# A fused attention and mixture-of-experts kernel: seven smaller expert weight loads, a later first load, and the last rank sums two slots later

## Chip, cores and metric

The kernel runs on one core of a Trainium2 chip. The metric is the device time of one execution in microseconds (us). KB are 1024 bytes.

## What is computed

The reference, cut to what matters:

```python
# 1. attention with decay, per batch and head; 3072 tokens of 384 = 8 heads x 48
for t in range(S):
    cur = einsum('bhd,bhe->bhde', u[None] * k[t], v[t])
    y[t] = einsum('bhd,bhde->bhe', r[t], state + cur)
    state = w * state + einsum('bhd,bhe->bhde', k[t], v[t])
# 2. dense layer, 384 -> 2048 -> 384
h = x @ w_in
x = (h * sigmoid(h)) @ w_out
# 3. eight experts, 384 -> 1024 -> 384; each token goes to one of them
e_idx = argmax(x @ w_gate + modality_bias[modality_id], axis=1)
gate_w = softmax(...)[e_idx]
for e in range(8):
    mask = e_idx == e
    out[mask] = gate_w[mask, None] * (maximum(x[mask] @ w1[e], 0) @ w2[e])
```

## The kernel before

All matrix products are done in three passes: each operand is split into a high and a low part (`_hi`, `_lo`, type float32r), and high x high, high x low and low x high are summed in PSUM. ScalarE makes the high parts (a cast), VectorE the low parts (a subtraction).

**Attention and dense stage.** `whole_block` writes out the program of every engine. The attention is cut into 48 units ("quads", u). The dense layer works on 12 tiles of 256 tokens; each has 16 *slots* f, one for every 128 of the 2048 inner features. In slot F = 16 t + f TensorE does the up step of f (`up_step`, nine matmuls, which raises `h_made`) and the down step of three slots before (`down_step`, six matmuls); the attention units are put into the slots by tables. The slots 0 to 2 of a tile have no down step of their own, since the tile before finished with them. In the last dense tile (t = 11, slots 176 to 191; F0 is 176) the first work for the experts is mixed in: `tensor_last_tile` transposes the gathered tokens of expert tile 0 in slot 3 (`turn`, L566 to L571, six transposes L570, waiting for `x_gathered`), `scalar_last_tile` makes the high parts of the first w1 in slots 8 to 11 and of the first w2 in slots 12 to 15, and `vector_last_tile` the low parts behind them.

**Expert stage.** Tokens are sorted by expert through lists in device memory. An expert tile is 256 tokens of one expert, and with these inputs there are 13 of them. In `tensor_experts` a tile has 8 up steps (nine matmuls each, L591 to L593), the down products of its first 128 tokens (8 x 3 matmuls, L618 to L620), the `turn` of the next tile's tokens, and the down products of the other 128 tokens. Tiles 0 and 1 are written out, the others run in a loop. In tile 0, VectorE chooses the experts of the last 512 tokens and counts them behind slot 1 (`route_choose`, `route_count`, L471 to L473); TensorE sums the ranks behind slot 3 (L595 to L601, waits for `lists_ready`); VectorE does the gates, takes the ranks and starts the tile table behind slots 4 to 6 (L474 to L485). At the end of tile 0 it computes the places, and GpSimd scatters the entries into the lists (L406 to L410).

**Weights.** An expert's w1 (128 x 3 x 1024, 1536 KB) goes to `raw1` and its w2 (128 x 8 x 384, 1536 KB) to `raw2`, each as one DMA from SyncE (`sync_load1`, `sync_load2`, L313 to L319). Each partition reads 12 KB in one piece. `raw1`, `raw2` and `x_in` lie in the buffer `store`, so the first load waits for the last attention unit (`y_done`). In SyncE's program the first load (`sync_first`) stands at slot 176, then the write of the tokens of dense tile 10 to `x_rows` (L896, waits for ScalarE's `copy_rows` in slots 0 and 1 of the last tile), then `sync_second` and the rest. A buffer is loaded again when the low parts have been made from it (`w1_lo_made`, `w2_lo_made`). The high and low parts of w2 lie in the first 8 rows of the dense layer's `wo_hi` and `wo_lo`, whose rows are 392 wide; 384 are used.

**GpSimd** (`pool_experts`) loads the list of the next tile (L989 for the first, then L358), gathers its tokens (L995 for the first, then L371, two indirect DMAs), and writes results out (L388, two indirect DMAs). Before it overwrites `entries_out` (L375), which ScalarE needs for the scales of the next results, it waits until the results written have landed.

## Time and profile before

| | |
|---|---|
| median of 3 runs | 782.63 us (782.56 to 784.86) |
| profiled execution, its time | 785.89 us |
| profiled execution, span | 784.3 us |
| TensorE busy | 743.2 us (95%) |
| VectorE, ScalarE, GpSimd busy | 501.8, 421.4, 235.0 us |
| mean granted clock of TensorE | 0.98 |
| DMA | 104.95 MB, mean 134 GB/s |
| last dense tile | about 501 to 540 us |
| expert tiles | about 540 to 774 us |

The profile is of one execution; times in it are from the start of its span. PE is TensorE's matmuls, PEld its weight loads, DVE VectorE, ACT ScalarE, POOL GpSimd, SP (SPq) SyncE. Engine clocks are given as a share of 2.4 GHz. A row of the windows view has the stretch and its length, the busy time (and number of instructions) of PE, PEld, DVE, ACT and POOL, the granted clock, the busy share of the DMA engines and GB/s. A row of a timeline has start, duration, engine, line, operation, output and inputs, and in brackets the idle time before it with what ended it. Matmuls overlap: each is shown with its whole passage, and the next starts before it ends (two up-step matmuls start about 0.12 us apart and take 0.28 each). "issue" as a releaser means that the view found no instruction that released the waiting one. Tiles that lie in the buffer `store` have its name in the rows (raw1, raw2, x_in); w1's parts are shown as wi_hi and wi_lo, w2's as wo_hi and wo_lo, and the experts' h likewise as wi_hi and wi_lo. in_w is w1 or w2 in device memory.

### The profile page before, as it was taken

To read this page: it belongs to the slowest core of one execution; us is meant where nothing else is said; L and a number is where in the kernel's file an instruction comes from. 1 tells how busy PE (TensorE), PEld (TensorE's weight loads), DVE (VectorE), ACT (ScalarE), POOL (GpSimd) and SP (SyncE) were. 2 spreads that over 40 slices of the span, in tenths; PEclk is the share of its full clock that TensorE was granted. 3 is DMA by queue.
4 is the path that set the end of the run, shared out by engine and by line. 5 is a ranking of instruction groups with operands and counts; after the bars stand their busy time and mean duration, and the time that the engine had idled before them with its cause. 6 is when DMAs were issued, how large, how long until landed. Compare 5 with 4: busy or idle time off the path is not lost.

```text
span 784.3 us, 24913 instructions
## 1 busy us (share of the span) xinstructions
PE 743.2 (95%) x9894; PEld 723.8 (92%) x9894; DVE 501.8 (64%) x1348; ACT 421.4 (54%) x1076; POOL 235.0 (30%) x349
## 2 busy tenths in 40 slices
PE   3599999999999999999999999899998999999994
PEld 3598899999999999999999999899998999999994
DVE  7889765856585666655676657245874766566662
ACT  4776555555453645555554554354563755566552
POOL 4531222332124222422133212210423334434431
PEclk9599999999999999999999999999999999999997
DMA  8941222222122222221222210505465755666561
GB/s 313 399 172 39 95 76 94 78 61 85 64 97 76 95 77 96 75 82 59 91 76 96 76 59 2 202 21 181 133 229 182 262 201 210 238 241 232 199 218 66
DMA packets 24160, 104.95 MB, mean 134 GB/s; under 512 B 4411, under 2 KB 9800, under 8 KB 20482
## 3 DMA queue, kind: packets, MB, share of 16 engines
q1 hardware_dynamic: 19362, 93.34, 33.5%
q0 software_dynamic: 4704, 10.29, 3.9%
q8 instruction: 68, 1.11, 0.6%
q14 instruction: 26, 0.21, 0.1%
HBM read 93.90 MB, written 10.11 MB: 133 GB/s over the span
## 4 chain that ended last, share of the span: by engine, by line
PE 76%; DVE 9%; issue 5%; DMA 4%; ACT 3%; POOL 1%; SPq 1%; POOLq 0%; ACTq 0%; DVEq 0%
PE ps_h L1471 8%; PE ps_h L1472 8%; PE ps_h L1473 8%; PE ps_o L1488 7%; PE ps_o L1489 6%; PE ps_o L1490 6%; PE ps_s L1415 5%; PE ps_o L618 4%; PE ps_o L620 4%; PE ps_o L619 4%; DVE x_lo L1247 2%; DVE state L1262 2%; PE ps_y L591 2%; PE ps_y L593 2%; PE ps_y L592 2%
## 5 line engine op out<-in xcount | busy, mean ns | idle before, releaser
L1072 ACT ACTIVATE g<-ps_h 128x256 f32<-128x256 f32 x192 | 73.5, 383 | 204.1 <-PE ps_h L1473 172.7
L1471 PE MATMUL ps_h<-x_hi,wi_hi 128*128 128x256 f32 x576 | 165.2, 287 | 5.3 <-DVE x_lo L1247 5.3
L1472 PE MATMUL ps_h<-x_lo,wi_hi 128*128 128x256 f32 x576 | 162.7, 282 | 0.0
L1473 PE MATMUL ps_h<-x_hi,wi_lo 128*128 128x256 f32 x576 | 162.3, 282 | 0.0
L1488 PE MATMUL ps_o<-wo_hi,g_hi 128*128 128x392 f32 x384 | 135.3, 352 | 2.7 <-DVE g_lo L1280 1.5
L1489 PE MATMUL ps_o<-wo_lo,g_hi 128*128 128x392 f32 x384 | 130.5, 340 | 0.0
L1490 PE MATMUL ps_o<-wo_hi,g_lo 128*128 128x392 f32 x384 | 130.5, 340 | 0.0
L942 POOL TENSOR_TENSOR store<-store,up_half 128x256 f32<-128x256 f32 x44 | 34.2, 776 | 312.4 <-PE ps_y L1458 310.9
L1280 DVE TENSOR_TENSOR g_lo<-g,g_hi 128x256 fp32r<-128x256 f32 x192 | 81.7, 428 | 65.1 <-ACT g_hi L1065 63.2
L1471 PEld LDWEIGHTS ps_h<-x_hi,wi_hi 128*128 128x128 f32 x576 | 110.2, 191 | 7.3 <-DVE x_lo L1247 5.5
L1473 PEld LDWEIGHTS ps_h<-x_hi,wi_lo 128*128 128x128 f32 x576 | 110.5, 192 | 0.0
L1472 PEld LDWEIGHTS ps_h<-x_lo,wi_hi 128*128 128x128 f32 x576 | 109.9, 191 | 0.0
L1247 DVE TENSOR_TENSOR x_lo<-ps_y,x_hi 64x256 fp32r<-64x256 f32 x132 | 55.5, 420 | 57.6 <-ACT x_hi L1040 55.5
L1065 ACT CAST g_hi<-g 128x256 fp32r<-128x256 f32 x192 | 78.0, 406 | 6.1
L1488 PEld LDWEIGHTS ps_o<-wo_hi,g_hi 128*128 128x128 f32 x384 | 72.1, 188 | 8.5 <-DVE g_lo L1280 6.3
L436 DVE TENSOR_TENSOR wo_lo<-store,wo_hi 128x768 fp32r<-128x768 f32 x52 | 49.4, 951 | 45.6 <-ACT wo_hi L515 45.6
L1489 PEld LDWEIGHTS ps_o<-wo_lo,g_hi 128*128 128x128 f32 x384 | 72.2, 188 | 0.0
L1490 PEld LDWEIGHTS ps_o<-wo_hi,g_lo 128*128 128x128 f32 x384 | 72.1, 188 | 0.0
L618 PE MATMUL ps_o<-wo_hi,wi_hi 128*128 128x384 f32 x208 | 71.4, 343 | 0.0
L620 PE MATMUL ps_o<-wo_hi,wi_lo 128*128 128x384 f32 x208 | 70.2, 338 | 0.0
L619 PE MATMUL ps_o<-wo_lo,wi_hi 128*128 128x384 f32 x208 | 70.1, 337 | 0.0
L1040 ACT CAST x_hi<-ps_y 64x256 fp32r<-64x256 f32 x132 | 48.1, 364 | 22.4 <-PE ps_y L1458 20.4
(205 smaller groups left out, 1606.4 us busy)
## 6 DMA issues: line engine op xcount, KB each, us to landing
store<-in_w SPq DMA_DIRECT2D x28, 1536.0 KB
store<-in_quads SPq DMA_DIRECT2D x48, 704.0 KB, 4.6
x_rows<-rows SPq DMA_DIRECT2D x12, 384.0 KB, 3.4
woT_raw<-in_woT SPq DMA_DIRECT2D x4, 768.0 KB, 10.1
wi_raw<-in_wi SPq DMA_DIRECT2D x4, 768.0 KB, 10.3
wo_raw<-in_wo SPq DMA_DIRECT2D x4, 768.0 KB, 11.8
store<-x_rows,entries POOLq DMA_INDIRECT x26
out_rows<-y,entries_out POOLq DMA_INDIRECT x26
```

What stands on the lines that cost most here:

```text
L618: T.matmul(o, hi, w2_hi[:, f, :], start=(f == 0), stop=False)
L619: T.matmul(o, hi, w2_lo[:, f, :], start=False, stop=False)
L620: last = T.matmul(o, lo, w2_hi[:, f, :], start=False, stop=(f == FCH - 1))
L1065: S.copy(g_hi[:, F % 4, :], g[:, F % 2, :]).then_inc(g_hi_made, 1)
L1072: S.activation(g[:, F % 2, :], ps_h[F % 2][:, 0:ETOK], ACT.Silu).then_inc(g_made, 1)
L1280: V.tensor_tensor(g_lo[:, F % 4, :], g[:, F % 2, :], g_hi[:, F % 4, :].bitcast(F32), ALU.subtract).then_inc(g_lo_made, 1)
L1471: T.matmul(out, hi, x_hi[:, t % 2, c, :], start=(c == 0), stop=False)
L1472: T.matmul(out, hi, x_lo[:, t % 2, c, :], start=False, stop=False)
L1473: last = T.matmul(out, lo, x_hi[:, t % 2, c, :], start=False, stop=(c == KC - 1))
L1488: T.matmul(out, hi, z.wo_hi[:, f, :], start=(f == 0), stop=False)
L1489: T.matmul(out, hi, z.wo_lo[:, f, :], start=False, stop=False)
L1490: last = T.matmul(out, lo, z.wo_hi[:, f, :], start=False, stop=(f == FCH - 1))
```

## The change

w1 is loaded in three DMAs of 128 x 1024 and w2 in four of 128 x 2 x 384, for every tile. `sync_first` is called after the loop over the slots, so behind the last write of `x_rows` in that loop. In the first load, each piece but the first of w1 waits for one more up step of the last dense tile. w2's high and low parts are packed without gaps. In expert tile 0, TensorE's rank sums move from slot 3 to slot 5, the reading of the ranks and the table sizes on VectorE to slot 6 and the table jumps to slot 7. The counts that ScalarE and SyncE wait for follow.

```diff
--- before.py
+++ after.py
@@ -252,7 +252,7 @@
 
     raw1, raw2, x_in = z.raw1, z.raw2, z.x_in
     w1_hi, w1_lo = (w[:, :, 0:z.F2] for w in (z.wi_hi, z.wi_lo))
-    w2_hi, w2_lo = (w[:, 0:FCH, 0:DM] for w in (z.wo_hi, z.wo_lo))
+    w2_hi, w2_lo = (w[:].rearrange("p f n -> p (f n)")[:, 0:FCH * DM].rearrange("p (f n) -> p f n", n=DM) for w in (z.wo_hi, z.wo_lo))
     xe_hi, xe_lo = (x[:, 0] for x in (front.x_hi, front.x_lo))
 
     def h_hi(f, at=0, n=ETOK):
@@ -310,42 +310,49 @@
         eng.wait_ge(table_made, 1)
         return eng.value_load(table[0:1, TABLE:TABLE + 1, 0:1], min_val=z.N // ETOK, max_val=z.ETILES)
 
-    def sync_load1(sp, tiles, j):
+    def sync_load1(sp, tiles, j, number):
         e = sp.value_load(tiles[0:1, bass.ds(j, 1), 0:1], min_val=0, max_val=E - 1)
-        sp.dma_start(raw1, w1_v[:, bass.ds(e, 1)].rearrange("p e c f -> p (e c) f")).then_inc(w1_in, 16)
+        for c in range(KC):
+            if number == 0 and c:
+                sp.wait_ge(front.h_made, F0 + c)
+            sp.dma_start(raw1[:, c], w1_v[:, bass.ds(e, 1), c].rearrange("p e f -> p (e f)")).then_inc(w1_in, 16)
         return e
 
-    def sync_load2(sp, e):
-        sp.dma_start(raw2, w2_v[:, bass.ds(e, 1)].rearrange("p e c d -> p (e c) d")).then_inc(w2_in, 16)
+    def sync_load2(sp, e, number):
+        for q in range(PIECES):
+            part2 = slice(q * FCH // PIECES, (q + 1) * FCH // PIECES)
+            if number == 0:
+                sp.wait_ge(front.h_made, F0 + KC + q)
+            sp.dma_start(raw2[:, part2], w2_v[:, bass.ds(e, 1), part2].rearrange("p e c d -> p (e c) d")).then_inc(w2_in, 16)
 
     def sync_first(sp):
         sp.wait_ge(front.table_made, 1)
         sp.wait_ge(front.y_done, QUADS)
-        sync_load2(sp, sync_load1(sp, z.first_tiles, 0))
+        sync_load2(sp, sync_load1(sp, z.first_tiles, 0, 0), 0)
 
     def sync_second(sp):
         sp.wait_ge(w1_lo_made, PIECES)
-        return sync_load1(sp, z.first_tiles, 1)
+        return sync_load1(sp, z.first_tiles, 1, 1)
 
     def sync_experts(sp, e):
         def tile(tiles, j):
 
             sp.wait_ge(w1_lo_made, PIECES * (j + 1))
-            e = sync_load1(sp, tiles, j + 1)
+            e = sync_load1(sp, tiles, j + 1, 2)
             sp.wait_ge(w2_lo_made, PIECES * (j + 1))
-            sync_load2(sp, e)
+            sync_load2(sp, e, 2)
 
         sp.wait_ge(w2_lo_made, PIECES)
-        sync_load2(sp, e)
+        sync_load2(sp, e, 1)
         tile(z.first_tiles, 1)
         tiles = tiles_with_tokens(sp)
         with sp.Fori(2, z.ETILES) as j:
             with sp.If(j < tiles):
                 tile(table, j)
         sp.sem_inc(sp_passed, 1)
-        sp.wait_ge(w1_in, 16 * (tiles + 1))
+        sp.wait_ge(w1_in, 16 * KC * (tiles + 1))
         sp.sem_inc(sp_passed, 1)
-        sp.wait_ge(w2_in, 16 * (tiles + 1))
+        sp.wait_ge(w2_in, 16 * PIECES * (tiles + 1))
         sp.sem_inc(sp_passed, 1)
         sp.wait_ge(y_out, 16 * EB * tiles)
         sp.sem_inc(sp_passed, 1)
@@ -474,14 +481,14 @@
                     if f == CHOICE_SLOT + 3:
                         dve.wait_ge(share_made, 1)
                         route_gate(nc, z, link)
+                    if f == CHOICE_SLOT + 5:
                         dve.wait_ge(ranks_ready, 1)
                         V.tensor_copy(ranks[:], ps_x[1][:, 1, 0:TB * E].rearrange("p (n e) -> p n e", e=E))
                         V.tensor_copy(t.n_of[:], ps_x[1][:, 1, TB * E:TB * E + E]).then_inc(ranks_read, 1)
                         dve.wait_ge(ranks_read, 1)
-                    if f == CHOICE_SLOT + 4:
                         dve.wait_ge(table_consts_made, 1)
                         table_sizes(nc, z, t, link, 2)
-                    if f == CHOICE_SLOT + 5:
+                    if f == CHOICE_SLOT + 6:
                         table_jumps(nc, z, t, link, 2)
                 if number == 1:
                     if f == 4:
@@ -523,10 +530,10 @@
         if f == 5:
             xe_high(act, 0)
         if 8 <= f < 8 + PIECES:
-            act.wait_ge(w1_in, 16)
+            act.wait_ge(w1_in, 16 * KC)
             w1_high(act, 0, f - 8)
         if f >= 12:
-            act.wait_ge(w2_in, 16)
+            act.wait_ge(w2_in, 16 * PIECES)
             act.wait_ge(front.f_summed, F0 + (f - 12 + 1) * FCH // PIECES)
             w2_high(act, 0, f - 12)
 
@@ -537,7 +544,7 @@
             for f in range(FCH):
                 if number > 0 and f < PIECES:
                     if f == 0:
-                        act.wait_ge(w2_in, 16 * (j + 1))
+                        act.wait_ge(w2_in, 16 * PIECES * (j + 1))
                         act.wait_ge(y_summed, j + 1)
                     w2_high(act, j, f)
                 act.wait_ge(h_made, FCH * j + f + 1)
@@ -546,7 +553,7 @@
                     act.wait_ge(below_made, 1)
                     nc.scalar.activation(z.share[:], z.below[:], ACT.Silu).then_inc(share_made, 1)
 
-            act.wait_ge(w1_in, 16 * (j + 2))
+            act.wait_ge(w1_in, 16 * KC * (j + 2))
             for q in range(PIECES):
                 w1_high(act, j + 1, q)
             xe_high(act, j + 1)
@@ -592,7 +599,7 @@
                     T.matmul(o, hi, xe_lo[:, c, :], start=False, stop=False)
                     last = T.matmul(o, lo, xe_hi[:, c, :], start=False, stop=(c == KC - 1))
                 last.then_inc(h_made, 1)
-                if number == 0 and f == CHOICE_SLOT + 2:
+                if number == 0 and f == CHOICE_SLOT + 4:
 
                     pe.wait_ge(lists_ready, 1)
                     rank_sums = ps_x[1][:, 1, 0:TB * E]
@@ -833,7 +840,7 @@
 
         front = type("Front", (), dict(
             x_hi=x_hi, x_lo=x_lo, rows=rows, ps_h=ps_h, ps_o=ps_o, ps_s=ps_s, ps_y=ps_y, y_done=y_done, att_made=att_made,
-            f_summed=f_summed, rows_made=rows_made, listed=listed, table_made=table_made, x_gathered=x_gathered))
+            f_summed=f_summed, h_made=h_made, rows_made=rows_made, listed=listed, table_made=table_made, x_gathered=x_gathered))
         experts = experts_stage(nc, z, A, out, sb, sem, front)
 
         block = ctx.enter_context(nc.Block())
@@ -894,8 +901,7 @@
                     t = F // FCH - 1
                     sp.wait_ge(rows_made, EB * (t + 1))
                     sp.dma_start(z.x_rows[t * ETOK:(t + 1) * ETOK, :].rearrange("(b p) d -> p b d", p=P), rows[:, t % 2, :, 0:DM]).then_inc(rows_out[t % 2], 16)
-                if F == FCH * (TILES - 1):
-                    experts.sync_first(sp)
+            experts.sync_first(sp)
             e = experts.sync_second(sp)
             sp.wait_ge(rows_made, EB * TILES)
             sp.dma_start(z.x_rows[(TILES - 1) * ETOK:TILES * ETOK, :].rearrange("(b p) d -> p b d", p=P), rows[:, (TILES - 1) % 2, :, 0:DM]).then_inc(rows_out[(TILES - 1) % 2], 16)
```

## Rows read from the trace of the kernel before

**Rows 1.** Windows view of one expert tile in the steady stage.
```profile
664.90:682.45 17.55, 17.55 (x128) 17.51 (x127) 11.08 (x18) 10.43 (x21) 6.82 (x8) 1.00 0.60 224
```

**Rows 2.** Waits view of TensorE: total us, times, longest.
```profile
PE ps_s L570 <- issue: 2.8, 1, 2.8
```

**Rows 3.** Timeline of TensorE around its waits.
```profile
507.04 1.51 PE L570 MATMUL ps_s<-ident,store 128*128 128x128 f32 x6 [2.79 <-issue]
...
510.24 0.34 PE L1488 MATMUL ps_o<-wo_hi,g_hi 128*128 128x392 f32 x1
...
543.11 0.28 PE L591 MATMUL ps_h<-x_hi,wi_hi 128*128 128x256 f32 x1
...
545.45 0.19 PE L599 MATMUL ps_s<-chosen,before 128*128 128x32 bf16 x1 [1.12 <-DVE earlier L92]
...
554.08 0.82 PE L570 MATMUL ps_s<-ident,store 128*128 128x128 f32 x6
...
590.67 0.88 PE L570 MATMUL ps_s<-ident,store 128*128 128x128 f32 x6 [1.33 <-DMA store<-x_rows,entries]
...
601.25 0.38 PE L591 MATMUL ps_y<-x_hi,wi_hi 128*128 128x256 f32 x1 [1.26 <-DVE wi_lo L466]
```

**Rows 4.** Windows view, the stretch behind the first wait.
```profile
507.00:510.30 3.30, 3.26 (x16) 3.29 (x17) 0.00 (x0) 0.00 (x0) 1.22 (x8) 0.52 0.07 17
```

**Rows 5.** Timeline of GpSimd, list loads, gathers and what waits for them.
```profile
495.25 0.76 POOL L989 DMA_DIRECT2D entries_next<-lists  x1 [4.93 <-issue]
500.77 0.99 POOL L995 DMA_INDIRECT store<-x_rows,entries_next  x1 [4.77 <-DMA entries_next<-lists]
...
508.23 0.75 POOL L358 DMA_DIRECT2D entries_new<-lists  x1 [5.21 <-issue]
...
510.58 0.18 POOL L363 COPY entries<-entries_new 128x4 int32<-128x4 int32 x1 [1.12 <-DMA entries_new<-lists]
...
515.04 0.98 POOL L371 DMA_INDIRECT store<-x_rows,entries  x1 [0.30 <-issue]
...
518.28 0.19 POOL L363 COPY entries<-entries_new 128x4 int32<-128x4 int32 x1 [1.71 <-DMA store<-x_rows,entries]
```

**Rows 6.** Timeline of SyncE: DMA issues.
```profile
495.57 0.35 SPq L315 DMA_DIRECT2D store<-in_w  x1
...
504.50 0.39 SPq L896 DMA_DIRECT2D x_rows<-rows  x1
```

**Rows 7.** Timeline of ScalarE, its first read of w1.
```profile
521.74 0.84 ACT L511 CAST wi_hi<-store 128x768 fp32r<-128x768 f32 x1
```

**Rows 8.** Windows view, the start of the kernel.
```profile
10.00:15.00 5.00, 2.66 (x103) 2.58 (x105) 5.00 (x13) 4.01 (x16) 3.77 (x6) 1.00 1.01 418
```

**Rows 9.** Timeline of VectorE, end of the count in expert tile 0.
```profile
544.64 0.75 DVE L92 TENSOR_TENSOR earlier<-earlier,chosen 128x8 bf16<-128x8 bf16 x4
```

**Rows 10.** The page, two groups of subtractions: busy us, mean ns, idle before.
```profile
L1280 DVE TENSOR_TENSOR g_lo<-g,g_hi 128x256 fp32r<-128x256 f32 x192 | 81.7, 428 | 65.1 <-ACT g_hi L1065 63.2
...
L436 DVE TENSOR_TENSOR wo_lo<-store,wo_hi 128x768 fp32r<-128x768 f32 x52 | 49.4, 951 | 45.6 <-ACT wo_hi L515 45.6
```

**Rows 11.** Timelines of SyncE and ScalarE, w2 in a steady tile.
```profile
674.58 0.33 SPq L319 DMA_DIRECT2D store<-in_w  x1
...
686.68 0.83 ACT L515 CAST wo_hi<-store 128x768 fp32r<-128x768 f32 x1
```

**Rows 12.** Chain that ended last, three transfers: start, us.
```profile
566.49 9.32 DMA lists<-entry,place
...
577.05 5.17 DMA entries_new<-lists
...
590.23 7.43 DMA out_rows<-y,entries_out
```

**Rows 13.** Timeline of GpSimd, a wait for a result write with no load beside it.
```profile
639.13 0.19 POOL L375 COPY entries_out<-entries_next 128x4 int32<-128x4 int32 x1 [1.78 <-DMA out_rows<-y,entries_out]
```

**Rows 14.** The page, a DMA issue: KB each, us to landing.
```profile
x_rows<-rows SPq DMA_DIRECT2D x12, 384.0 KB, 3.4
```

## The prediction

> **What bounds the kernel now.** I read the windows view first, for the steady stage. In one expert tile (664.90 to 682.45) TensorE is busy for all 17.55 us at a granted clock of 1.00, while VectorE has 11.08 and ScalarE 10.43 [rows 1]. The kernel is bound by TensorE's matmuls there, and nothing in the change removes a matmul. So a gain can only come out of the places where TensorE stands still, and I looked for these in the waits view, whose longest of TensorE in the second half of the span is 2.8 us before the transposes of L570 [rows 2]. The timeline of TensorE places it and shows three more: 1.12 us before the rank sums of L599, 1.33 before L570 again in tile 2, and 1.26 before an up step of the experts (L591) at 601.25 [rows 3].
>
> **First place: the turn in slot 3 of the last dense tile.** TensorE's last matmul before it ends at 504.25 (507.04 less 2.79). Back to back the next would have started some 0.16 us earlier, at 504.1. The down step of that slot starts at 510.24 [rows 3]. Between lie six transposes and one up step. At full clock six transposes take 0.82 us with their tail, about 0.6 to the next start (the row at 554.08), and an up step takes 1.06 us: slot 3 of expert tile 0 starts at 543.11, and 545.45 less 1.12 less the tail of 0.16 is 544.17. So 6.15 us went by for 1.66 us of work: a loss of 4.5 us, of which 2.8 is the wait. The remaining 1.65 is the clock: granted 0.52 from 507.00 to 510.30 [rows 4], which is the 1.2 GHz level, after TensorE had stood for 2.8 us.
>
> Why it waits: GpSimd loads the first list (L989) at 495.25 and gets it only at 500.77, then issues two gathers, and x arrives at about 507. SyncE had issued both expert loads, 3 MB, from 495.57 on [rows 5, 6]. Without such a load beside it, the same kind of list load takes at most 2.35 us (508.23 to 510.58), and two gathers land at most 2.3 us after the second has been issued (515.04 + 0.98 to 518.28) [rows 5].
>
> After the change: the first load stands behind the write of x_rows in SyncE's program, and that write waits for rows copied by ScalarE in slot 1; it is issued at 504.50 [rows 6]. So no weights move before 504.9. The list lands at 495.25 + 2.35 = 497.6, the gathers are issued by 497.6 + 0.99 + 0.30 + 0.98 = 499.9, x is there at 502.2, and TensorE asks at 504.1: 1.9 us to spare. I take the whole 4.5 us in the profiled execution. The **pacing** itself does little: at 504.9 three up steps of the tile are finished, so the three w1 pieces and the first w2 piece go out in a row, and only the last three w2 pieces (up steps 4, 5, 6) wait. What works is the later start.
>
> What the later start may cost: ScalarE first reads w1 at 521.74 [rows 7], in the new time 517.2. From 505, 3.1 MB of weights and 0.4 MB of the second gather at the 418 GB/s that many queued loads reached at the start of the kernel [rows 8] need 8.5 us, so all has landed by about 514. Cover 3 us; were it gone, ScalarE would hold back the Silu of slot 8 and TensorE with it, by what is missing. The second gather (it collides with this burst) is wanted only at the turn of expert tile 0, 40 us later. SyncE has nothing else queued: behind the paced pieces comes the second w1 load, at 530.71 before. Cost taken: 0, bounds 0 and +1.
>
> **Second place: the ranks, two slots later.** In expert tile 0 VectorE's choice and count begin behind slot 1 and end at 545.39 (544.64 + 0.75) [rows 9]; TensorE wants them behind slot 3, at 544.17, and gets to go at 545.45. Behind slot 5 it arrives at 544.17 + 2 x 1.06 = 546.3, 0.9 us after they are ready: 1.2 us gained. What is late next: slot 6 needs h_lo of slot 2, which VectorE makes right behind the count, by 545.7, before 546.4. VectorE's rank copies and the table sizes (7 small operations of about 0.2 us) move behind slot 6 and the jumps behind slot 7, so that the low halves of the next w1 start about when they did before, measured from TensorE's work; these have 2 us of cover before tile 1. Cost 0, bounds 0 and +0.5. The wait for ranks_read at the second half of the down products comes 4 us later still.
>
> **w2 rows side by side.** Removes gaps of 8 elements from the copies, subtractions and matmul operands. VectorE's 768-element subtraction takes 951 ns on gapped rows, and 256 contiguous elements take 428 [rows 10]: 1.02 ns an element for the 512 between them, so the gaps cost nothing now. 0; bounds -0.1 us a tile at best, inside cover.
>
> **Seven smaller loads a tile.** Each extra issue costs SyncE 0.34 us, plus some 0.1 of register work: the last w1 piece starts about 0.9 us later, the last w2 piece 1.4. SyncE only waits otherwise. In the steady stage w2 is issued at 674.58 and first read at 686.68 [rows 11]: 12.1 us for 1.5 MB. Cover is large if the pieces overlap.
>
> **Third place: tile 2.** The two other waits come from one chain on GpSimd [rows 12]: the last scatter of the ranks takes 9.32 us from its start (some 1.0 of them GpSimd's own issue, so 8.3 behind it), the list load behind it 5.17, the gather is late by 1.33 us for TensorE at 589.3, and the result write of tile 1 takes 7.43 us, so that ScalarE gets its scales late and TensorE waits 1.26 us at 601 [rows 3]. Each of the three transfers has a weight load beside it. Without one the scatter was done within 4.93 us behind its issue (the wait before L989) and a list load within 2.35 [rows 5], and a result write 1.8 us behind its issue of 1.0 [rows 13]. So the chain carries some 3.4 + 2.8 + 4.6 us of contention, and 1.5 us less ends the first wait; an earlier gather also sends the result write out before the w1 load of 590.71, which ends the second. A weight load is now 128 rows of 12 KB, 8 for each of the 16 DMA engines; afterwards these are 24 of 4 KB or 32 of 3 KB, so a small transfer that takes turns with it stands behind 3 or 4 KB each time, not 12. Bounds: 0 (the share of the engines is what counts, not the size) and -3.0 us (both waits and the restarts behind them). I take -2.9, since half of the contention in the scatter alone (1.7) would do.
>
> The Trainium skill's page "DMA: Bandwidth & Descriptors", section "Queues, rings and completion order", says that an engine takes turns between its queues at packet granularity. By that rule the third part is -2.9; if turns were by bytes it would be 0.
>
> **Sum against the profiled execution** (785.89, span 784.3): -4.5 -1.2 -2.9 = -8.6, 777.3. The median of the three runs is 3.3 us lower than that execution, and they spread by 2.3 themselves. I read this as the clock having fallen in some executions and not in others, since 2.8 us of standing still is one chance for it. For the median I therefore count the first place as 2.8: 782.63 - 2.8 - 1.2 - 2.9 = 775.7.
>
> **Rivals.**
> - *Contention stays* (0.25): packets' size doesn't matter, the waits of tile 2 stay. For it: nothing in this trace shows one small transfer beside loads of two sizes. 782.63 - 4.0 = 778.6, or 777 with the clock part.
> - *The stall is mostly the profiler's* (0.07): the median runs, 3.3 us faster, hardly have the first one. Then 782.63 - 1.2 - 0.5 = 780.9, which can't be told from no change. Against: 3 MB queued ahead of a gather don't depend on a profiler.
> - *Slower* (0.04): the pieces follow one another with a landing time each, in place of overlapping. A transfer of 384 KB lands in 3.4 us [rows 14]; four in a row are 13.6 us against the 12.1 of cover for w2, 1.5 us late in each of 12 tiles: 782.63 + 18 - 6.9, so 794. It decides once a piece costs over 3 us on its own. Against: loads of 0.7 MB queued together moved 418 GB/s [rows 8].
>
> The skill's same page, section "Bandwidth", wants DMAs of 1 MiB and more for 75% of peak; with its fit of 2.0 us fixed each, four serial pieces would be an estimated 11.6 us, just inside that cover.
>
> **Numbers.** All three parts 0.62, at 775.7; 0.02 for a new wait I don't see. A measurement here can tell about 0.3% from no change, 2.35 us, so faster means under 780.3. Low end 773.5: all parts in full with the clock part in the median runs too (774.0). High end 779.5, past the first rival with an up to 1 us late first load. Faster 0.89, same 0.07, slower 0.04.
>
> **What would show it.** Right: SyncE's first weight issue just behind x_rows at about 504.9, no wait before L570 in slot 3, the clock at 1.00 there, no wait before L599, the scatter landing in about 6 us in place of 8.2, and no waits of TensorE in tile 2. Wrong: ScalarE waiting for w1 at slot 8 or for w2 in a steady tile, TensorE waiting for h_lo in slots 6 and 7, an expert tile longer than 17.55 us, or the scatter as long as before.

## The result, and the profile after

The changed kernel took 773.96 us (median of 3 runs, 772.99 to 776.71) against 782.63 before: a ratio of 0.9872, with a 95% interval of 0.9843 to 0.9901. That is faster: 8.7 us by the two medians, 10.0 by the ratio (0.0128 x 782.6), where 6.9 were forecast. The median lies in the range of 773.5 to 779.5; taken by the ratio the time would be 772.6, just under its low end. The sum behind the forecast was wrong in two places: one part that was costed at nothing gave 4.5 to 4.9 us, and one that was to give 2.9 gave little or nothing.

The profiled execution of after took 776.71 us (span 775.1, against 784.3). **First the windows view** of a steady expert tile, and of the two stretches around the turn in slot 3 of the last dense tile:

```profile
658.32:675.49 17.17, 17.17 (x128) 17.14 (x127) 11.04 (x18) 10.43 (x22) 6.61 (x8) 1.00 0.66 229
...
504.10:507.00 2.90, 2.90 (x25) 2.90 (x24) 0.85 (x2) 2.06 (x6) 1.01 (x9) 1.00 0.40 136
507.00:510.30 3.30, 3.30 (x26) 3.30 (x25) 0.85 (x2) 1.00 (x3) 1.78 (x2) 1.00 0.84 267
...
586.00:588.00 2.00, 1.66 (x9) 1.66 (x10) 0.00 (x0) 0.55 (x2) 0.37 (x2) 0.72 0.83 284
588.00:590.20 2.20, 2.20 (x9) 2.20 (x8) 1.02 (x2) 0.79 (x3) 0.19 (x1) 0.50 1.01 410
```

The first row answers to [rows 1]: TensorE is busy for the whole tile, at the same granted clock of 1.00 and with the same number of matmuls, but the tile takes 17.17 us and not 17.55. The second and third answer to [rows 4]: where TensorE had stood still and then run at 0.52, it is busy throughout at 1.00. The last two show where the fallen clock is now, behind a wait in tile 2.

**The timeline of TensorE**, against [rows 3] (the lines of the code have moved: L570 is L577, L591 is L598, L599 is L606, L1488 is L1494, L618 is L625):

```profile
504.50 0.82 PE L577 MATMUL ps_s<-ident,store 128*128 128x128 f32 x6
...
506.19 0.34 PE L1494 MATMUL ps_o<-wo_hi,g_hi 128*128 128x392 f32 x1
...
542.25 0.19 PE L606 MATMUL ps_s<-chosen,before 128*128 128x32 bf16 x1
...
586.34 1.08 PE L577 MATMUL ps_s<-ident,store 128*128 128x128 f32 x6 [3.05 <-DMA store<-x_rows,entries]
...
588.17 0.52 PE L625 MATMUL ps_o<-wo_hi,wi_hi 128*128 128x384 f32 x1
588.49 0.52 PE L626 MATMUL ps_o<-wo_lo,wi_hi 128*128 128x384 f32 x1
...
661.49 0.28 PE L598 MATMUL ps_y<-x_hi,wi_hi 128*128 128x256 f32 x1
...
662.50 0.28 PE L598 MATMUL ps_y<-x_hi,wi_hi 128*128 128x256 f32 x1
...
669.64 0.34 PE L625 MATMUL ps_o<-wo_hi,wi_hi 128*128 128x384 f32 x1
...
673.82 0.82 PE L577 MATMUL ps_s<-ident,store 128*128 128x128 f32 x6
...
678.66 0.28 PE L598 MATMUL ps_y<-x_hi,wi_hi 128*128 128x256 f32 x1
```

From the turn's start to the down step 1.69 us go by; before it was 6.15 with the wait. The rank sums start without a wait. The turn of tile 2 waits 3.05 us, longer than the 1.33 before, and at the clock of 0.50 behind it down matmuls start 0.32 us apart. The wait at an up step in the next tile (601.25 in [rows 3]) is gone. The last five rows are from one steady tile: its first and its second up step, its first down matmul, its turn, and the first up step of the next tile. The same rows of before, also in the timeline of TensorE:

```profile
668.43 0.28 PE L591 MATMUL ps_y<-x_hi,wi_hi 128*128 128x256 f32 x1
...
669.49 0.28 PE L591 MATMUL ps_y<-x_hi,wi_hi 128*128 128x256 f32 x1
...
676.91 0.34 PE L618 MATMUL ps_o<-wo_hi,wi_hi 128*128 128x384 f32 x1
...
681.13 0.82 PE L570 MATMUL ps_s<-ident,store 128*128 128x128 f32 x6
...
685.99 0.28 PE L591 MATMUL ps_y<-x_hi,wi_hi 128*128 128x256 f32 x1
```

One up step of nine matmuls takes 1.01 us and not 1.06. All eight take 8.15 and not 8.48, the first half of the down products 4.18 and not 4.22, the turn and the second half 4.84 and not 4.86. So most of the 0.38 us comes from the up steps, which don't read w2.

**The whole difference of the spans** comes out of the starts of the tiles' first up steps. Tile 0 starts 4.05 us earlier (535.88 against 539.93): the 4.5 of the first place less 0.4 by which this execution was later when it came to slot 3. From start to start tile 0 takes 17.61 and not 19.01, tile 1 17.18 and not 17.55, tile 2 22.12 and not 19.10, tile 3 17.18 and not 19.47, tile 4 17.17 and not 17.55, tile 5 17.17 and not 18.27, and the seven from tile 6 on 0.38 less each. That is -4.05 - 1.40 - 0.37 + 3.02 - 2.29 - 0.38 - 1.10 - 2.66 = -9.2, the difference of the spans. In tile 5 before had lost 0.72 us, with a short wait for VectorE's low parts (0.25 at 640.67). The prediction had no term for it; the same loss is in e1 below and not in e2, e3 or e4, so which part ended it in after isn't shown.

**The chain that ended last** (start, us) against [rows 12]:

```profile
561.03 6.87 DMA lists<-entry,place
...
569.14 5.83 DMA entries_new<-lists
...
579.13 7.16 DMA store<-x_rows,entries
```

The scatter is 2.45 us shorter than the 9.32 before. The list load is not shorter, and a gather is now the third link, where it was a result write. **The timeline of SyncE** says what these three lie beside:

```profile
504.91 0.38 SPq L903 DMA_DIRECT2D x_rows<-rows  x1
506.44 1.43 SPq L318 DMA_DIRECT2D store<-in_w  x3
507.98 3.21 SPq L326 DMA_DIRECT2D store<-in_w  x4
...
559.68 5.00 SPq L326 DMA_DIRECT2D store<-in_w  x4
569.09 1.37 SPq L318 DMA_DIRECT2D store<-in_w  x3
577.45 1.88 SPq L326 DMA_DIRECT2D store<-in_w  x4
```

The scatter runs beside the w2 pieces of 559.68, the list load beside the w1 pieces of 569.09, the gather beside the w2 pieces of 577.45. The first weights go out behind x_rows, as forecast, 1.5 us later than forecast. ScalarE's first read of them is at 517.69, without a wait on them, so that this cost nothing. The page of the profile has the packets of all DMAs at 34240 (24160 before).

### The profile page after: what moved, and what is told of

It is laid out like the page before. It is cut to its first block, busy times and chain, and to the rows that moved or that the text cites. A ratio compares the mean times of both kernels' runs of the same rounds, so it can differ in the third digit from the quotient of the medians.

```text
span 775.1 us, 25124 instructions
## 1 busy us (share of the span) xinstructions
PE 737.7 (95%) x9894; PEld 719.4 (93%) x9894; DVE 501.8 (65%) x1348; ACT 421.8 (54%) x1076; POOL 235.3 (30%) x349
## 2 busy tenths in 40 slices
DMA packets 34240, 104.96 MB, mean 135 GB/s; under 512 B 5531, under 2 KB 10920, under 8 KB 34146
## 4 chain that ended last, share of the span: by engine, by line
PE 79%; DVE 10%; issue 4%; DMA 3%; ACT 2%; POOL 1%; POOLq 0%; ACTq 0%; DVEq 0%
PE ps_h L1477 8%; PE ps_h L1478 8%; PE ps_h L1479 8%; PE ps_o L1494 7%; PE ps_o L1495 6%; PE ps_o L1496 6%; PE ps_s L1421 5%; PE ps_o L625 4%; PE ps_o L626 4%; PE ps_o L627 4%; DVE x_lo L1253 2%; DVE state L1268 2%; PE ps_h L598 2%; PE ps_y L598 2%; PE ps_y L599 2%
## 5 line engine op out<-in xcount | busy, mean ns | idle before, releaser
L1494 PE MATMUL ps_o<-wo_hi,g_hi 128*128 128x392 f32 x384 | 135.5, 353 | 2.7 <-DVE g_lo L1286 1.5
L1494 PEld LDWEIGHTS ps_o<-wo_hi,g_hi 128*128 128x128 f32 x384 | 72.1, 188 | 8.5 <-DVE g_lo L1286 6.3
L625 PE MATMUL ps_o<-wo_hi,wi_hi 128*128 128x384 f32 x208 | 71.6, 344 | 0.0
```

The source lines that it names most:

```text
L625: T.matmul(o, hi, w2_hi[:, f, :], start=(f == 0), stop=False)
L1494: T.matmul(out, hi, z.wo_hi[:, f, :], start=(f == 0), stop=False)
```

## The experiments

All ratios are to the kernel before, run on the same chip. The medians are those of one group of runs each, so the ratio and not the difference of two medians of different groups is what compares; its intervals reach 0.13 to 0.3% to either side. In these groups before has medians of 785.0 to 785.6, and not the 782.63 of its first three runs.

### The parts alone

Three questions: does each part give what the sum said, and where do the 0.38 us a tile come from? The theory was that w2's rows side by side do it; the rivals were the new order of the ranks, the later first load, and the smaller loads.

**e1_ranks**, the ranks alone:

```diff
-                if number == 0 and f == CHOICE_SLOT + 2:
+                if number == 0 and f == CHOICE_SLOT + 4:
```

(and VectorE's reading of the ranks, table sizes and jumps moved as in the change).

> The kernel before with the ranks moved alone (TensorE's rank sums to slot 5, VectorE's reading to slots 6 and 7). All theories: no wait before the rank sums, -1.2 us. Theory A (the experts' up-step matmuls start 113 ns apart in place of 118 since the rank sums run without a wait at slot 5): an expert tile of 17.17 us, in all -6 us. Theories B (the packed w2 does it) and C (the smaller pieces do it): 17.55 us a tile, in all -1.2 us.

Median 784.16 against 785.58, ratio 0.9984 (0.997 to 0.9997). The wait before the rank sums is gone, the steady tile takes 17.55 us.

**e2_late**, the first load behind the loop, alone, unsplit and without pacing:

```diff
-                if F == FCH * (TILES - 1):
-                    experts.sync_first(sp)
+            experts.sync_first(sp)
```

> The kernel before with the first load behind the slot loop alone (two DMAs, no pacing). All theories: list load and gathers of expert tile 0 undisturbed, no wait before the turn in slot 3 of the last dense tile and no fallen clock there: -2.8 us where the clock had held, -4.5 where it had fallen. Expert tiles 17.55 us. If the pacing were needed, a wait before the turn of expert tile 0 or ScalarE late with w1 would show.

Median 782.03 against 785.58, ratio 0.9952 (0.9938 to 0.9966), so -3.8 us (-2.7 to -4.9). The windows view of this kernel, the same stretches as in [rows 4]:

```profile
504.10:507.00 2.90, 2.90 (x24) 2.90 (x23) 1.00 (x3) 1.56 (x5) 0.22 (x2) 1.00 0.74 200
507.00:510.30 3.30, 3.30 (x26) 3.30 (x25) 0.43 (x1) 1.17 (x3) 2.29 (x3) 1.00 0.83 329
```

No wait and no fallen clock: the later start alone does the first place. It lies between the 2.8 (wait) and the 4.5 (wait and clock) of the prediction, and its interval takes in both. Tiles take 17.55.

**e3_packed**, w2's parts side by side, alone:

```diff
-    w2_hi, w2_lo = (w[:, 0:FCH, 0:DM] for w in (z.wo_hi, z.wo_lo))
+    w2_hi, w2_lo = (w[:].rearrange("p f n -> p (f n)")[:, 0:FCH * DM].rearrange("p (f n) -> p f n", n=DM) for w in (z.wo_hi, z.wo_lo))
```

> The kernel before with w2's parts packed alone. Theory B (the packing makes the experts' matmuls start closer together): an expert tile of 17.17 us, -4.9 us. Theories A and C: no difference (within 0.3 us), 17.55 us a tile.

Median 781.55 against 785.58, ratio 0.9938 (0.9912 to 0.9965), so -4.9 us (-2.7 to -6.9). The windows view of a steady tile:

```profile
663.24:680.41 17.17, 17.17 (x127) 17.14 (x126) 11.03 (x19) 10.44 (x20) 6.83 (x8) 1.00 0.62 229
```

17.17, as in after, with nothing else changed. Eleven tiles of 0.38, with 0.18 in tile 0 and 0.09 in tile 1, make 4.45 us in the trace, inside the interval. The three rivals fall, as each of the other three parts alone left the tile at 17.55.

**e4_split**, seven loads a tile, alone, unpaced, the first where it was:

```diff
-        sp.dma_start(raw1, w1_v[:, bass.ds(e, 1)].rearrange("p e c f -> p (e c) f")).then_inc(w1_in, 16)
+        for c in range(KC):
+            sp.dma_start(raw1[:, c], w1_v[:, bass.ds(e, 1), c].rearrange("p e f -> p (e f)")).then_inc(w1_in, 16)
```

(w2 likewise in four).

> The kernel before with seven loads a tile alone, the first where it was and not paced. Theory C (smaller pieces disturb TensorE's reads less): an expert tile of 17.17 us, -4.9 us. Theories A and B: 17.55 us. For the small transfers of tile 2: if turns are taken by packet, the scatter lands in about 7 us in place of 9.3, the list load is no shorter, and the gather is longer where it meets the w2 load; the wait before the turn in the last dense tile stays at 2 to 4 us.

Median 785.0 against 785.58, ratio 0.9978 (0.9954 to 1.0001): at most a little gained. TensorE's timeline:

```profile
507.38 1.51 PE L573 MATMUL ps_s<-ident,store 128*128 128x128 f32 x6 [2.59 <-issue]
...
591.50 0.77 PE L573 MATMUL ps_s<-ident,store 128*128 128x128 f32 x5 [2.06 <-DMA store<-x_rows,entries]
```

Smaller pieces don't help the first gather past 3 MB of weights. In tile 2 the wait at the turn grows to 2.06 and the one in tile 3 is gone. The list load is issued at 574.96, not 577.05, so the scatter was sooner done, and that did not bring the gather in.

The four ratios multiply to 0.985, and after has 0.987 (0.9843 to 0.9901): within the intervals the parts don't depend on each other.

### What of the packing makes the matmuls faster

Packing does three things: rows are 384 elements apart (1536 bytes) and not 392 (1568), the gap is gone, and rows start at other addresses. Kernels with nothing changed but the distance and the start of the rows tell these apart. The line of e3 was used with another number (and for all distances but 384 ScalarE waits for one to four down steps more before it overwrites rows in the dense layer's last tile), for e5:

```diff
-[:, 0:FCH * DM].rearrange("p (f n) -> p f n", n=DM)
+[:, 0:FCH * 400].rearrange("p (f n) -> p f n", n=400)[:, :, 0:DM]
```

**e5_pitch400**: 400 elements, 1600 bytes, 25 x 64.

> The kernel before, w2's parts still with gaps, but rows 400 elements apart (1600 bytes, a multiple of 64) in place of 392 (1568 bytes, only every other row start on a multiple of 64). Theory D (what counts is where a row that TensorE streams begins, modulo 64 bytes): an expert tile of 17.17 us, -4.9 us. Theory E (the gap itself, that is rows that don't follow one another, costs): 17.55 us, no difference.

Median 786.1 against 785.49, ratio 1.0009 (0.9991 to 1.0026). The windows view of a steady tile shows the slow pace:

```profile
664.54:682.12 17.58, 17.58 (x127) 17.55 (x126) 11.07 (x19) 10.44 (x20) 6.81 (x8) 1.00 0.61 224
```

Rows that start on multiples of 64 bytes are not it.

**e6_shift8**: packed as in e3, all of it begun 8 elements (32 bytes) later.

> The kernel before with w2's parts packed without gaps, but the whole block begun 8 elements (32 bytes) later. Theory D: every row starts 32 bytes off, so 17.55 us a tile or more, no gain. Theory E: 17.17 us a tile, -4.9 us.

Median 782.22 against 785.49, ratio 0.9966 (0.9948 to 0.9985); the tile takes 17.16 us (658.67 to 675.83). So a start 32 bytes later doesn't matter, the distance does. The reading rests on the tile: the median gained 2.7 us (1.2 to 4.1), less than the 4.9 of e3, though the two intervals overlap.

**b2_pitch512** and **b3_pitch448**: rows 2048 and 1792 bytes apart, with gaps of 128 and 64 elements, one execution each.

> The kernel before with w2's rows 512 elements apart (gaps of 128, all row starts the same modulo 512 bytes and modulo 2048). Theory H (the row starts must agree modulo a power of two of at least 128 bytes, as with 384 elements): an expert tile of 17.17 us. Theory E (rows must follow one another without a gap): 17.55 us or more.

> The kernel before with w2's rows 448 elements apart (1792 bytes: the same modulo 256 bytes, not modulo 512). Theory H with 256 bytes or less: 17.17 us a tile; H with 512 bytes, or theory E: 17.55 us.

780.95 and 781.73 us, tiles of 17.17 (660.89 to 678.06) and 17.18 (661.71 to 678.89). A gap is harmless. What 384, 448 and 512 elements have in common, and 392 and 400 don't, is a whole multiple of 256 bytes.

**b6_pitch416**: 1664 bytes, 13 x 128, one execution.

> The kernel before with w2's rows 416 elements apart (1664 bytes, 13 x 128). If row starts have to agree modulo 128 bytes: an expert tile of 17.17 us; if modulo 256: 17.55 to 17.6 us.

782.39 us; the windows view of a tile:

```profile
661.65:678.93 17.28, 17.28 (x127) 17.24 (x126) 11.05 (x19) 10.44 (x20) 6.81 (x8) 1.00 0.62 228
```

And in the timeline of TensorE one tile of it, the rows that were shown for before and after:

```profile
666.53 0.28 PE L591 MATMUL ps_y<-x_hi,wi_hi 128*128 128x256 f32 x1
...
674.71 0.34 PE L618 MATMUL ps_o<-wo_hi,wi_hi 128*128 128x384 f32 x1
...
678.93 0.82 PE L570 MATMUL ps_s<-ident,store 128*128 128x128 f32 x6
...
683.81 0.28 PE L591 MATMUL ps_y<-x_hi,wi_hi 128*128 128x256 f32 x1
```

17.28: nearly, but not quite. The eight up steps take 8.18 us, nearly the 8.15 of after. The down products stay where they were in before: 4.22 for the first half, 4.88 for the turn and the second. So two things hang on the distance, and a multiple of 128 bytes gave only the gain of the up steps, which is the larger one.

**b4_dense512**: after, with the dense layer's own rows (392 wide, in `wo_hi`, `wo_lo`) 512 elements apart, and the buffers they are loaded to likewise, to see whether its 12 tiles could have the same gain.

```diff
-    z.wo_hi = sb(dense, "wo_hi", [P, F1 // P, z.DM + E], F32R)
+    z.wo_hi = sb(dense, "wo_hi", [P, F1 // P, 512], F32R)
```

> The kernel after with the dense layer's wo_hi and wo_lo 512 wide in place of 392 (392 columns used). Theory H: the dense stage's matmuls start closer together (up steps 113 ns in place of 117 to 118, so up to 1728 x 4 ns = 7 us), the version would beat both kernels. Theory E: the rows of 392 that followed one another now have gaps, so the dense stage is the same or slower.

Median 774.56 against 785.15, ratio 0.9855 (0.9833 to 0.9877), not to be told from after. In the traces the dense stage gained a little: from one write of `x_rows` to the next 41.49 us (mean of the six tiles from 218.26 to 467.21), where before has 41.68 and after 41.66 for the same six. That is 0.2 us a tile and at most some 2 us in all, where up to 7 had been expected. And in expert tile 0, whose up steps follow on the dense layer's down steps, the up-step matmuls before the rank sums start 0.114 to 0.116 us apart, which are 0.1175 to 0.119 apart in all the other kernels; the tile takes 17.38 us and not 17.61. So the distance counts there too, but for little.

### Tile 2: why the split gave so little

The theory from the profile of after: the scatter gains from small packets, but what it gains is lost by the next two transfers, which meet the w1 and the w2 pieces. The rival: the split gains what was forecast, and another part of the change cost something in tile 2.

**e7_unsplit**: after with one load each and no pacing (ranks, late load and packing in). **a0_after**: after again, in the same group of runs.

```diff
-        for c in range(KC):
-            sp.dma_start(raw1[:, c], w1_v[:, bass.ds(e, 1), c].rearrange("p e f -> p (e f)")).then_inc(w1_in, 16)
+        sp.dma_start(raw1, w1_v[:, bass.ds(e, 1)].rearrange("p e c f -> p (e c) f")).then_inc(w1_in, 16)
```

> The kernel after with one load for each of w1 and w2 again and no pacing (late first load, ranks moved and packing kept). Theory F (the smaller pieces give nothing, they only move the waits of tile 2 from the result write to the gather): within 0.2% of the kernel after; tile 2 waits 1.1 to 1.8 us for its gather and tile 3 about 1.2 us for VectorE, as before. Theory G (the pieces help by freeing the small transfers): 2 us slower than the kernel after.

> The kernel after, once more, in more rounds and beside the others. If the parts add up: ratios of the four single parts 0.9984 x 0.9952 x 0.9938 x 0.9978 = 0.985 of the kernel before, 11.6 us less; by its first three runs 0.987.

Medians 776.47 and 775.29 against 785.49, ratios 0.989 (0.9873 to 0.9908) and 0.9871 (0.9849 to 0.9893): the split's share is 1.2 us, less than these intervals tell. The chain that ended last, of e7:

```profile
560.96 11.19 DMA lists<-entry,place
...
573.39 3.62 DMA entries_new<-lists
```

And the same view of a0:

```profile
560.65 6.81 DMA lists<-entry,place
...
568.70 4.75 DMA entries_new<-lists
...
578.22 6.65 DMA store<-x_rows,entries
```

The scatter takes 11.19 us beside 12 KB rows and 6.81 beside 3 KB pieces: the mechanism of the prediction is right for it. The other kernels bear this out: the transfer takes 9.32 to 11.19 us beside whole loads (before, e1, e2, e3, e5, e6, e7, b2, b3, b6) and 6.81 to 7.91 beside pieces (after, a0, b1, b4, b8, e4). The 9.32 of before, from which the prediction reckoned, is the shortest of its kind. But then the list load, whose w1 load was issued at 569.0 or 568.7 in both kernels, takes 4.75 and not 3.62, because it comes right on top of that load and not 4 us behind it. And the gather, second half issued at 578.22 in a0 and at 581.28 in e7, lands at 584.91 and 585.11. Both had their w2 load issued at 577.0 or 577.5. So of the 4.4 us gained by the scatter 0.2 are left at the gather, and a0's scatter had begun 0.3 earlier. With its second half issued 1.2 us behind the first w2 piece, the gather takes some 6.7 us in a0; issued 3.8 us behind the w2 load, it takes 3.83 in e7 and 3.59 in before (587.08 to 590.67). TensorE's wait for it is 1.83 in e7, 2.04 in a0. Tiles 2 and 3 together take 38.29 us in e7 and 38.27 in a0.

**b1_gather_first** tests that: in tile 2 alone, the w2 load waits for the gather.

```diff
             sp.wait_ge(w2_lo_made, PIECES * (j + 1))
+            if first:
+                sp.wait_ge(x_gathered, 16 * EB * (j + 1))
             sync_load2(sp, e, 2)
```

> The kernel after, with one more wait on SyncE: the w2 load that is issued in tile 2 (for tile 3) waits until tile 2's gather has landed. Theory K (the gather of tile 2 lands late because it shares the DMA engines with that w2 load, whatever its pieces): the gather lands about 3.5 us after its second issue in place of 7, no wait before the turn of tile 2, no fallen clock there; 2 to 4 us less than the kernel after. Rival (the gather is late by its own queue): no difference. w2 starts 4 to 5 us later and is read 15 us after its issue now, so no wait on it.

Median 774.05 against 785.15, ratio 0.9844 (0.9821 to 0.9867). The chain that ended last:

```profile
561.04 7.91 DMA lists<-entry,place
...
570.19 6.25 DMA entries_new<-lists
...
581.26 3.81 DMA store<-x_rows,entries
```

With no load beside it the gather takes 3.81 from the issue of its second half and not 6.65 or 7.16, as expected. (In e7 and before, where it came 3.8 us behind the load, it was as short.) But the list load took 6.25 beside the w1 pieces this time, so the gather was issued later and the wait stayed (1.81). One transfer was freed and the one before it held the chain up. The expectation of no wait on w2 failed as well: ScalarE waited 0.24 us for it at 592.29, and tile 3 took 18.27 us and not 17.17.

**b5_lists_first** and **b7_lists_first_unsplit**: the w1 load that is issued in tile 2 waits for the list load as well, in after and in e7. (Tile 2 is written out in front of SyncE's loop for this, here and in b1.)

```diff
             sp.wait_ge(w1_lo_made, PIECES * (j + 1))
+            if first:
+                sp.wait_ge(entries_in, 16 * (j + 1))
```

> The kernel after with two waits on SyncE in tile 2: the w1 load for tile 3 waits for the list load, the w2 load for tile 3 for the gather. Theory K (small transfers are late by the loads beside them, so the order of issue decides): the list load takes 2.4 us in place of 5 to 6, the gather lands before TensorE asks, no wait in tiles 2 and 3, both of 17.2 to 17.4 us: 3.5 to 4 us less than the kernel after. Rival (the scatter before them is the whole delay): the wait before the turn of tile 2 stays above 1 us.

> The same two waits in the kernel after with one load each for w1 and w2 and no pacing. If the pieces matter only through the scatter (which landed 4 to 5 us sooner beside pieces): list load started at 573 again, gather just late, a wait of 0 to 1 us before the turn of tile 2, so 0 to 1.5 us slower than b5. If pieces don't matter at all: equal to b5.

b5: median 772.64 against 785.0, ratio 0.9847 (0.9832 to 0.9862). b7: 773.96, ratio 0.9866 (0.985 to 0.9882). The profiled executions took 771.05 and 771.03. The timeline of TensorE of b5:

```profile
582.11 0.34 PE L632 MATMUL ps_o<-wo_hi,wi_lo 128*128 128x384 f32 x1
582.29 0.82 PE L582 MATMUL ps_s<-ident,store 128*128 128x128 f32 x6
582.86 0.42 PE L630 MATMUL ps_o<-wo_hi,wi_hi 128*128 128x384 f32 x1
```

And of the same kernel the timeline of GpSimd:

```profile
568.60 0.76 POOL L370 DMA_DIRECT2D entries_new<-lists  x1 [5.74 <-issue]
571.09 0.18 POOL L375 COPY entries<-entries_new 128x4 int32<-128x4 int32 x1 [1.73 <-DMA entries_new<-lists]
...
575.38 0.99 POOL L383 DMA_INDIRECT store<-x_rows,entries  x1 [0.30 <-issue]
...
581.39 0.81 POOL L387 COPY entries_out<-entries_next 128x4 int32<-128x4 int32 x1 [2.35 <-DMA out_rows<-y,entries_out]
```

The list load takes 2.49 us to the next instruction, the result write holds GpSimd for 2.35 (3.56 in after, 3.38 in a0), and TensorE doesn't wait at the turn of tile 2 nor after it. b7 is the same without the split: its scatter is slow (GpSimd stood 9.09 us before the list load), and still TensorE shows no wait; ScalarE waits 2.8 us for the w1 load that was held back, which TensorE doesn't feel. Tiles 2 and 3 together take 34.46 us in b5 and 34.63 in b7, against 38.27 in a0. So it is the order in which SyncE issues, not the size of the pieces, that ends the waits of tile 2. Whether the pieces are worth the 1.3 us between the medians of b5 and b7 can't be told: the intervals overlap.

**b8_no_pace**: after without the waits for up steps in the first load.

```diff
-            if number == 0 and c:
-                sp.wait_ge(front.h_made, F0 + c)
```

(and the one before the w2 pieces).

> The kernel after without the waits on up steps in the first load. All theories: no difference (within 0.3%), no wait before the turn of the last dense tile, and ScalarE not late with w1 or w2.

Median 774.81 against 785.0, ratio 0.986 (0.9832 to 0.9888), no wait in slot 3 of the last dense tile. The pacing does nothing that can be measured.

## Why the prediction was right and wrong

**First place, right.** The whole 4.5 us are gone in the profiled execution: the wait, and the clock of 0.52 behind it. In the medians the late load alone is worth 3.8 (2.7 to 4.9), which doesn't tell the 2.8 that I counted there from the 4.5. My ground for the 2.8 doesn't hold: the first median of before lay 3.3 under the profiled execution, but in the four later groups before has medians of 785.0 to 785.6, so that the 785.89 was an ordinary execution. And of the nine profiled kernels that still wait at this turn (2.12 to 2.98 us), the clock fell behind the wait in eight (0.50 to 0.71 over the next 3 us) and stayed at 1.00 in one (e6, 2.19 us). The reason for the gain held, as did the remark that the later start does it and the pacing doesn't (e2, b8). The first issue at 506.44 and not 504.9, and the first read at 517.69 with no wait, bear out the cost of 0.

**Second place, right.** -1.2 forecast, 0.9984 (-1.25, with an interval of -0.2 to -2.4) measured, and no wait before the rank sums.

**w2 rows side by side, wrong.** The step that failed: "1.02 ns an element for the 512 between them, so the gaps cost nothing now. 0". I priced the gaps by VectorE's reading of them, and took it that what is left is "inside cover". VectorE indeed didn't change (952 ns for the subtraction, 951 before). The matmuls did. w2's parts are an operand of the down products, these stand in the stage that TensorE bounds, and I hadn't asked what their distance does to TensorE. Nor had the sum a bound for it: -0.1 us a tile was the best I allowed, and 0.38 came in each tile from the third on, 4.5 us in the trace and 4.9 (2.7 to 6.9) in the medians. A rival "the layout of a matmul operand is part of its price" was missing. The steady expert tiles of before have one pace, at a granted clock of 1.00, and nothing in them says whether that is the floor. The dense layer of the same trace did hint at it: its up-step matmuls, of the same shape and at the same clock, start 0.115 us apart in some slots (eight gaps from 515.54 to 516.46) and 0.1175 in others (513.43 to 514.37). That asked for a bound on the gain side.

**Third place, wrong in its end, half right in its mechanism.** The failed step: "Bounds: 0 ... and -3.0 us ... I take -2.9, since half of the contention in the scatter alone (1.7) would do". The scatter did give up more than that, 2.45 in after and 4.4 between e7 and a0. What I left out is that the transfers behind it have loads of their own beside them, and move onto them when they come earlier: the list load meets the w1 pieces, the gather the w2 pieces. I had treated the contention of the three as a store from which any part could be taken. Tile 2 and tile 3 together took +3.02 - 2.29 = +0.7 us, although the packing took 0.8 off them, and in the medians the split is worth 0 to 1.7 (e4 alone 1.7, with an interval that takes in nothing; e7 against a0 1.2, less than their intervals tell). The wait of 1.26 us in tile 3 did end, as forecast: the last result write is issued at 582.48 and the w1 load behind it at 584.71, 2.2 us apart where there were 0.5 before (590.23 and 590.71). In e7 that issue comes 0.4 behind the w1 load (585.08 and 584.69), and there TensorE still waits 0.89 us in tile 3.

The Trainium skill, page "DMA: Bandwidth & Descriptors", section "Queues, rings and completion order", says that an engine takes turns between its queues at packet granularity. For the scatter the runs agree (6.81 against 11.19 us). The third part's -2.9, which I drew from it, doesn't follow: a rule on one transfer isn't one on a chain.

**The rivals.** "Contention stays" came nearest for tile 2, for another reason than the one it gave. "The stall is mostly the profiler's" fell with e2. "Slower, serial pieces" fell: ScalarE waits for no weight in any tile of after, a piece of w2 takes 4.5 us from issue to landing by the page of the profile and still four of them, issued within 1.88 us, come in time, and e4 isn't slower than before. The Trainium skill, same page, section "Bandwidth", asks for DMAs of 1 MiB and more; loads of 384 and 512 KB queued together cost nothing here.

So by the runs the sum is -3.8 (late load), -1.25 (ranks), -4.9 (packing) and 0 to -1.7 (split): -10 to -11.7 by parts, against -10 for the whole by both its ratios (0.9872 and 0.9871), -8.7 by the medians of the first timing. The forecast's size was near by luck: 4.9 not forecast and most of 2.9 not received partly made up for each other.

**The version without a wait in tile 2** is b5, after with the two waits of SyncE there: 0.9847 (0.9832 to 0.9862), against 0.9871 (0.9849 to 0.9893) for after in a0, timed in another group. The intervals overlap, and b1 has 0.9844 (0.9821 to 0.9867) with its wait, so that b5 is faster than after or b1 isn't shown by the medians; that tile 2 has no wait is shown.

**Still open.** Why the up steps, which don't read w2, get faster as well (0.118 to 0.113 us a matmul). In after this sets in only at the rank sums of tile 0. What the runs show is that the slow pace outlasts the down steps that come before: ahead of the rank sums of tile 0 those are the dense layer's, with rows 392 apart, and only in b4, with 512, are the up steps there fast. The rank sums can end it: in e1, e4 and e5, with w2's rows 392 or 400 apart, the up steps behind them ran at 0.1125 to 0.114, and fell back in tile 1 (e4, e5) or tile 2 (e1); in before and e2 they didn't. So the distance is not all that sets the pace, and what carries it from one step to the next isn't known. Not tried: splitting w1 alone or w2 alone, and holding w2 of the tile before back for the scatter.

## What to carry to other kernels

Where TensorE bounds a stage, the distance of the rows of its moving operand belongs in the sum: try a multiple of 256 bytes (it gave 2.2% of the expert tiles here and 0.5% of the dense tiles), and compare the pace of a steady stretch, not only its waits. When a chain of small transfers runs beside large loads, a faster first link can just move the next one onto the next load, as here; ask for each link what lies beside it at its new time, and let the large load wait for the small one where TensorE asks for the small one first. Splitting and pacing loads were worth little here; starting the first one later was worth 3.8 us (2.7 to 4.9).

## What was not expected of the hardware

- The matmuls of an expert tile took 17.17 us with w2's rows 384, 448 or 512 elements of 4 bytes apart, 17.28 with 416, and 17.55 to 17.58 with 392 or 400, at a granted clock of 1.00 in all of them. A start 32 bytes later changed nothing.
- Up matmuls, which don't read those rows, went from 117.8 to 113.3 ns (means of seven undisturbed tiles), and the down matmuls of a tile's first half, which do, from 175.7 to 173.9. With rows 416 apart the up matmuls had 113.6 and the down ones 175.8.
- Beside GpSimd's scatter, SyncE needed 5.00 us to issue four pieces (559.68), where it took 1.88 otherwise (577.45). It was the same in a0, b1, b4, b5 and e4: 4.52 to 4.98 us beside the scatter.
- Behind a wait at a turn the clock fell in some executions and not in others: it was 0.50 in after behind 3.05 us, 0.69 on the mean of 585 to 590.5 in a0 behind 2.04, and stayed at 1.00 in b4_dense512 behind 2.31 and in e6 behind 2.19. That explains little of the 5 to 6 us by which executions of before spread in the two large groups: those with a mean granted clock of 0.99 took 785.2 us on average, those with 0.98 785.9.
